# Top-32 attention, soft and top-2 mixture of experts: the first of three strikes of the search moved to ScalarE and TensorE, tiles of a pair staggered

## What is computed

```python
batch, n_heads, seq, head_dim = (4, 8, 576, 64)
scores = scale * np.matmul(q, k.transpose(0, 1, 3, 2))
kth = np.partition(scores, -top_k, axis=-1)[..., -top_k:-top_k + 1]   # top_k = 32
mask = scores >= kth
scores = np.where(mask, scores, -1000000000.0)
scores = scores - np.max(scores, axis=-1, keepdims=True)
attn = np.exp(scores)
attn = attn / (np.sum(attn, axis=-1, keepdims=True) + 1e-09)
return np.matmul(attn, v).astype(np.float32)
```

## Time and profile before

| | |
|---|---|
| runs | 1154.96, 1158.04, 1158.5 us; median 1158.04 |
| the profiled execution | 1157.69 us, of which the span of the instructions is 1155.9 us |
| busy in the span | TensorE 933.9, VectorE 877.4, GpSimd 651.5, ScalarE 416.3 us |
| first and last score search on VectorE | from 7.2 us to about 707.7 us |
| mean granted clock of TensorE | 0.855 of full speed |

### The profile page before, as it was taken

How to read it: one execution, slowest core, us unless ns; L and a number is a source line. 1 busy time by engine, 2 the same in 40 slices (tenths; PEclk the granted TensorE clock), 3 DMA queues, 4 the chain that set the end, 5 groups by cost and what they waited for, 6 DMA issues and landing times.

```text
span 1155.9 us, 18485 instructions
## 1 busy us (share of the span) xinstructions
PE 933.9 (81%) x5335; PEld 721.3 (62%) x5335; DVE 877.4 (76%) x1813; ACT 416.3 (36%) x767; POOL 651.5 (56%) x812
## 2 busy tenths in 40 slices
PE   4777878778888777787777888775779999999995
PEld 3666666566666666666666667322347877778884
DVE  7999999999999999999999996302754344543431
ACT  3444444444444444444444443101244122331110
POOL 2777777777777777777777775100214344444442
PEclk7878787887778888888888787886779999999998
DMA  9811010010010010010110000889923344433232
GB/s 357 354 43 41 3 43 19 23 42 19 23 42 6 37 42 9 33 42 0 42 42 5 37 0 1 321 362 421 425 124 67 83 111 112 111 39 39 39 44 33
DMA packets 21581, 105.06 MB, mean 91 GB/s; under 512 B 2944, under 2 KB 4016, under 8 KB 12464
## 3 DMA queue, kind: packets, MB, share of 16 engines
q1 hardware_dynamic: 13696, 84.53, 18.6%
q0 software_dynamic: 7136, 11.20, 7.4%
q10 hardware_dynamic: 720, 8.98, 2.1%
HBM read 88.35 MB, written 16.07 MB: 90 GB/s over the span
## 4 chain that ended last, share of the span: by engine, by line
issue 39%; DVE 27%; PE 25%; DMA 5%; DVEq 1%; ACT 1%; POOL 1%; SPq 0%; POOLq 0%; ACTq 0%
PE psum L742 11%; DVE arena L913 8%; DVE arena L917 8%; DVE arena L906 5%; PE psum L747 5%; DMA arena<-xs_rows,arena 3%; DMA arena<-w_soft 2%; PE psum L731 2%; PE psum L639 1%; DVE w_lo L1108 1%; PE psum L713 1%; DVE arena L932 1%; PE psum L532 1%; PE psum L620 1%; DVE arena L1083 1%
## 5 line engine op out<-in xcount | busy, mean ns | idle before, releaser
L913 DVE MATCH_REPLACE8 arena<-arena 128x576 f32<-128x576 f32 x432 | 320.2, 755 | 0.0
L917 DVE MAX8 arena<-arena 128x8 f32<-128x576 f32 x432 | 307.4, 760 | 0.0
L499 PE MATMUL psum<-arena 128*128 128x128 f32 x576 | 129.1, 364 | 154.4 <-POOL arena L1197 154.4
L1191 POOL TENSOR_SCALAR arena<-arena 128x576 bf16<-128x576 f32 x142 | 244.6, 1731 | 6.6
L484 PE MATMUL psum<-arena 128*128 128x288 f32 x576 | 220.4, 545 | 4.2 <-DMA arena<-qkv 4.2
L512 PEld LDWEIGHTS psum<-arena 128*128 128x128 f32 (+3 forms) x1600 | 193.4, 182 | 29.7 <-issue 3.3
L512 PE MATMUL psum<-arena 128*128 128x65 f32 (+3 forms) x1600 | 207.4, 271 | 0.9 <-ACT arena L786 0.9
L499 PEld LDWEIGHTS psum<-arena 128*128 128x128 f32 x576 | 81.6, 179 | 186.9 <-POOL arena L1197 161.4
L484 PEld LDWEIGHTS psum<-arena 128*128 128x128 f32 x576 | 152.1, 278 | 52.5 <-DMA arena<-qkv 4.2
L1197 POOL TENSOR_TENSOR arena<-arena 128x576 f32<-128x576 f32 x142 | 178.5, 1278 | 0.0
L785 ACT COPY arena<-psum 128x512 f32<-128x512 f32 x144 | 84.3, 586 | 233.8 <-PE psum L500 233.8
(11 more groups left out here) (177 smaller groups left out, 950.8 us busy)
## 6 DMA issues: line engine op xcount, KB each, us to landing
weights<-w_soft SPq DMA_DIRECT2D x21, 1024.0 KB, 17.3
arena<-qkv SPq DMA_DIRECT2D x15, 1189.0 KB, 5.1
weights<-w_top SPq DMA_DIRECT2D x12, 1024.0 KB, 27.3
arena<-w_soft SPq DMA_DIRECT2D x11, 1024.0 KB, 10.9
weights<-w_top SPq DMA_DIRECT2D x3, 2048.0 KB, 20.9
weights<-w_top ACTq DMA_DIRECT2D x3, 2048.0 KB, 7.7
out<-arena SPq DMA_DIRECT2D x1, 4864.0 KB, 18.4
arena<-w_top SPq DMA_DIRECT2D x4, 1024.0 KB, 27.6
```

The source lines that it names most:

```text
L499: nc.tensor.transpose(bank(4 + t % 2, P, c * P), src[:, c * P:(c + 1) * P], ident)
L913: nc.vector.match_replace(work[t % 2], m8[t % S_SLOTS][:, 8 * r - 8:8 * r], src, NEG) \
L917: nc.vector.max(m8[t % S_SLOTS][:, 8 * r:8 * r + 8], work[t % 2]) \
L1191: nc.gpsimd.tensor_scalar(keep[t % 2], s_sb[t % S_SLOTS], m8[t % S_SLOTS][:, TOPK - 1:TOPK], None, ALU.is_ge) \
```

## The change

For each tile:
- VectorE does four MAX8 and two MATCH_REPLACE8. The first strike is gone from it: ScalarE computes `above` = relu(8th largest - score) from PSUM (bf16), then `hit` = relu(1 - 2^100 * above), which is 1 where a score is at least the 8th largest and 0 elsewhere, and its row sum `n_hit`. Both lie in the tile's `e_sb`, which the exponentials fill later. TensorE then adds hit times -2^126 to the scores in PSUM with two bf16 matmuls (`strike`, weights: the identity times -2^126).
- The second MAX8 and the second strike read those struck scores in PSUM. So the banks of a tile stay in use until that strike (`struck16`), and `qk` of tile t+2 waits for that and no more for the copy.
- With ties the first strike can remove more than 8 scores. So the 32nd value is taken by the count: `sat` is min(n_hit, 32) (a VectorE operation on 128x1), and `select` picks among 25 columns of `m8` the one that belongs to it (an operation on 128x25 with a sum), into `kth_sb`, which the masks now read.
- `qk` contracts 64 partitions: the queries of a head stand in both halves of the partitions, half x holds the keys 288x to 288x+287, and the two matmuls use the two halves of the array's rows. The odd tile takes four matmuls of 64 queries in place of two of 128.
- The work of tiles a and b is listed apart, so that they run half a step shifted, and part of the search of duo n now runs in step n+1. GpSimd's masks run up to a step later.

```diff
+            def qk(j, n, x_, t):
...
+                (pe.wait_ge if w < 2 * NC else partial(hold, pe))(struck16, TPI * j + t + 1)
+                for h, q0, rows in ((w // NC, 0, P),) if w < 2 * NC else ((0, 0, REM), (1, REM, REM)):
                     for x in range(2):
-                        last = nc.tensor.matmul(bank(2 * (t % 2) + x, SH), qT[u][:, w * P:(w + 1) * P],
-                                                kT[u][:, x * SH:(x + 1) * SH], start=True, stop=True)
-                    last.then_inc(scores, 1)
+                        half = slice(HD * x, HD * x + HD)
+                        last = nc.tensor.matmul(bank(2 * (t % 2) + x, SH)[q0:q0 + rows, :],
+                                                qT[u][half, w * P + q0:w * P + q0 + rows],
+                                                kT[u][half, h * SH:(h + 1) * SH], start=True, stop=True,
+                                                skip_group_check=True)
+                last.then_inc(scores, 1)
+            def strike(j, n, x_, t):
...
+                pe.wait_ge(copied, TPI * j + t + 1)
+                pe.wait_ge(hits, TPI * j + t + 1)
+                for x in range(2):
+                    last = nc.tensor.matmul(bank(2 * (t % 2) + x, SH), strike_w, hit[t % S_SLOTS][:, x * SH:(x + 1) * SH],
+                                            start=False, stop=True, skip_group_check=True)
+                last.then_inc(cut, 1)
...
-            steps(pe, [(0, qk), (LAG_O, attn_v), (LAG_T, trans)], lambda m: a_work(early_tiles(m)))
+            steps(pe, [(0, qk_a), (1, strike_b), (LAG_O, attn_v), (0, qk_b), (0, strike_a), (LAG_T, trans)], lambda m: a_work(early_tiles(m)))
...
+            def find_hits(j, n, x, t):
...
+                act.wait_ge(transp, TPI * j + t + 1)
+                act.wait_ge(top8, TPI * j + t + 1)
+                nc.scalar.activation(by_half(above[t % S_SLOTS]), scores_of(t), ACT.Relu,
+                                     bias=m8[t % S_SLOTS][:, 7:8], scale=-1.0).then_inc(relus, 1)
+                act.wait_ge(relus, TPI * j + t + 1)
+                nc.scalar.activation(hit[t % S_SLOTS], above[t % S_SLOTS], ACT.Relu, bias=ones[:, 0:1], scale=STEEP,
+                                     accum_out=n_hit[:, t % S_SLOTS:t % S_SLOTS + 1]).then_inc(hits, 1)
...
-            steps(act, [(0, copy_scores), (LAG_E, exps), (LAG_O, copy_o), (LAG_T, copy_wt)],
+            steps(act, [(0, copy_a), (LAG_E, exp_a), (0, hits_a), (LAG_O, copy_o),
+                        (0, copy_b), (LAG_E, exp_b), (LAG_T, wt_a), (0, hits_b), (LAG_T, wt_b)],
                   lambda m: xT_even(early_tiles(m)))
...
+            def second8(j, n, x, t):
+                hold(dve, cut, TPI * j + t + 1)
+                nc.vector.max(top(t, 1), scores_of(t)).then_inc(top16, 1)
+            def strike16(j, n, x, t):
+                hold(dve, top16, TPI * j + t + 1)
+                nc.vector.match_replace(by_half(work[t % 2]), top(t, 1), scores_of(t), NEG).then_inc(struck16, 1)
...
+            def fourth8(j, n, x, t):
+                slot = t % S_SLOTS
+                nc.vector.tensor_scalar(n_sat[:, slot:slot + 1], n_hit[:, slot:slot + 1], float(TOPK), None,
+                                        ALU.min).then_inc(saturated, 1)
+                hold(dve, struck24, TPI * j + t + 1)
+                nc.vector.max(top(t, 3), work[t % 2]).then_inc(top32, 1)
+            def select(j, n, x, t):
+                slot = t % S_SLOTS
+                dve.wait_ge(saturated, TPI * j + t + 1)
+                hold(dve, top32, TPI * j + t + 1)
+                nc.vector.scalar_tensor_tensor(chosen[x], cst[:, C_KTH:C_KTH + PICKED], n_sat[:, slot:slot + 1],
+                                               m8[slot][:, 7:TOPK], ALU.is_equal, ALU.mult,
+                                               accum_out=kth_sb[:, slot:slot + 1]).then_inc(kth, 1)
...
-            steps(dve, [(0, search_first), (0, search_rest), (LAG_E, mask_last), (LAG_O, recips)],
+            steps(dve, [(1, second_b), (0, first_a), (1, s24_a), (1, s16_b), (1, fourth_a), (1, third_b), (1, select_a),
+                        (0, second_a), (0, first_b), (1, s24_b), (0, s16_a), (LAG_O, recips), (1, fourth_b), (0, third_a),
+                        (1, select_b), (LAG_E, mask_last)],
                   lambda m: xT_odd(early_tiles(m)))
...
-            steps(pool, [(0, neg_max), (LAG_O, o_sums), (LAG_E, mask), (LAG_O, norm)])
+            steps(pool, [(2, mask_b), (2, apply_a), (2, apply_b), (LAG_O, o_sums), (1, mask_a), (0, neg_max), (LAG_O, norm)])
```

More of the change, by code:

```diff
@@ L14 @@
 from contextlib import ExitStack
+from functools import partial
 import concourse.bass as bass
@@ L46 @@
 NEG = -3.0e38
+STRIKE = -2.0 ** 126
+STEEP = -2.0 ** 100
 N, D = B * S, H * HD
@@ L72 @@
 C_BACK = C_LOW + 1
-CW = C_BACK + 1
+C_KTH = C_BACK + 1
+PICKED = TOPK - 7
+CW = C_KTH + PICKED
 M_SAME = 0
@@ L166, in build @@
         zeros = take(D)
+        above = [a[:, 0:S // 2].bitcast(BF16) for a in e_sb]
+        hit = [a[:, S // 2:S].bitcast(BF16) for a in e_sb]
+        strike_w = tiny.bitcast(BF16)
+        n_hit, n_sat, kth_sb = [pos[:, a * S_SLOTS:(a + 1) * S_SLOTS] for a in range(3)]
+        chosen = [list_f[:, a * PICKED:(a + 1) * PICKED] for a in range(2)]
         (w3, wgn_f, so_sb, more, part, slotP_f, ed_f, sm, noise_sb, logit_f, cT_f, soT_f, so4_f, sow, rt_f,
@@ L762, in _ @@
             act.sem_inc(av, 1)
[L764 to L772, removed]
@@ new lines, in exps, with copy_wt @@
+            def exps(j, n, x, t):
+                act.wait_ge(negmax, DPI * j + n + 1)
+                act.wait_ge(copied, TPI * j + t + 1)
+                act.wait_ge(cut, TPI * j + t + 1)
+                nc.scalar.activation(e_sb[t % S_SLOTS], s_sb[t % S_SLOTS], ACT.Exp,
+                                     bias=nmax[n % 3][:, x:x + 1], scale=SCALE).then_inc(expd, 1)
+            def copy_wt(j, n, x, t):
+                if x == 0:
+                    act.wait_ge(av, DPI * j + n + 1)
+                act.wait_ge(transp, TPI * j + t + 1 + S_SLOTS)
+                last = nc.scalar.copy(wT[:, t % 2, 0:NC, :], bank(4 + t % 2).rearrange("p (c q) -> p c q", c=NC))
+                if x == 1:
+                    last = nc.scalar.copy(wT[0:REM, :, NC, :], bank(6, 2 * P)[0:REM, :].rearrange("p (t q) -> p t q", t=2)) \
+                        .then_inc(wt_copied, 1)
@@ L1215, in norm @@
                 last.then_inc(x_done, 1)
-            steps(pool, [(0, neg_max), (LAG_O, o_sums), (LAG_E, mask), (LAG_O, norm)])
+            mask_a, mask_b = each(mask)
+            apply_a, apply_b = each(apply)
+            steps(pool, [(2, mask_b), (2, apply_a), (2, apply_b), (LAG_O, o_sums), (1, mask_a), (0, neg_max), (LAG_O, norm)])
             pool.wait_ge(zeroed, 32)
@@ L1322 @@
     qt = q.transpose(0, 1, 3, 2).reshape(PAIRS, 2, HD, S)
-    for w in range(2 * NC):
-        h, c = w // NC, w % NC
-        qkv[:, HD * h:HD * (h + 1), w * P:(w + 1) * P] = qt[:, h, :, c * P:(c + 1) * P]
-    for h in range(2):
-        first = 2 * NC * P + REM * h
-        qkv[:, HD * h:HD * (h + 1), first:first + REM] = qt[:, h, :, NC * P:S]
-    qkv[:, :, QW:QW + S] = k.transpose(0, 1, 3, 2).reshape(PAIRS, P, S)
+    for x in range(2):
+        rows = slice(HD * x, HD * x + HD)
+        for h in range(2):
+            qkv[:, rows, h * NC * P:(h + 1) * NC * P] = qt[:, h, :, 0:NC * P]
+            first = 2 * NC * P + REM * h
+            qkv[:, rows, first:first + REM] = qt[:, h, :, NC * P:S]
+    kt = k.transpose(0, 1, 3, 2).reshape(PAIRS, 2, HD, 2, SH)
+    qkv[:, :, QW:QW + S] = kt.transpose(0, 3, 2, 1, 4).reshape(PAIRS, P, S)
     vp = v.reshape(PAIRS, 2, S, HD)
```

123 lines of the change are left out of this document (70 added, 53 removed).

## The result

| | before | after |
|---|---|---|
| runs | median 1157.15 us of 4 (1154.96 to 1158.5) | median 1218.72 us of 4 (1218.48 to 1221.98) |
| ratio to before, 95% interval | | **1.0541** [1.0515, 1.0566] |
| profiled execution, span | 1157.69, 1155.9 us | 1221.98, 1220.2 us |
| mean granted clock | 0.855 | 0.774 |
| last full-width search operation ends | 707.7 us | 768.4 us |

The search ends 60.7 us later; behind it, 3.6 us more pass than before. Rather than a forecast gain of 44 us there is a loss of 62.

The account below looks back on a forecast made before the run. VectorE's list was taken to bound the attention: 9.70 - 1.44 + 0.44 + 0.35 = 9.05 us a duo. Over 72 duos 47 us less, 3 more for the ends: 1157.7 - 44 = 1114 us, range 1086 to 1148.

Parts of the forecast that it names:

- TensorE's loop: Strike, hand-overs, scores and second MAX8 in attention: 4.2 us each half duo, 8.4 a duo, below 9.05; clock 0.8 or more.
- the slow rival: Attention paced by the loop through TensorE at low clock: 9.8 us a duo, 1168 us, up to 1219; chance 0.14.
- two hand-overs: Between VectorE and TensorE in each half duo: 0.12 us each, partly an estimate.
- List on VectorE: VectorE's own work in attention: 9.70 - 1.44 + 0.44 = 8.70 us a duo; alone, as a rival, 1089 us, chance 0.22.
- PSUM as source at no cost: Four VectorE operations a duo reading PSUM: cost 0, bounds 0 and 0.045 us an operation; dearer as a rival, chance 0.03.
- `select` waits for GpSimd: On VectorE, `select` has two SBUF inputs and waits for GpSimd's operations: 0.35 us for tile a, 0 for b.
- `sat` waits: Rival on VectorE: `sat` waits too, 0.35 us a duo more, 9.40 a duo, 1139 us; chance 0.15.
- ScalarE hidden: Four more 128x576 passes on ScalarE, 3.1 us a duo, 7.5 of 9.05 in all: hidden by the search, costed at nothing.
- The row halves run side by side: Score matmuls on TensorE's array halves: half the time, 0.53 us a tile; rival of one after the other, chance 0.08.
- The mark set for being wrong: Profile sign: VectorE idle before the second MAX8, released by TensorE, means the loop paces; clock under 0.75, the slow case.

Follow-up runs that it names:

- e2: Kernel before the change with only the scores changed to half height (64 partitions a matmul, two row halves): 1155.76 us, ratio 0.9989.
- e1: Changed kernel with the old full-height scores (128 partitions with zeros, one matmul after the other): 1219.75 us, ratio 1.0534.
- e3: Changed kernel with four of five matmuls of `attn_v` left out, so the output is incomplete: 1179.80 us, ratio 1.0193.
- e7: Changed kernel with six dummy bf16 matmuls of 512 columns a step on TensorE, behind the transposes: 1148.21 us, ratio 0.9914.
- e9: Kernel before the change with 108 semaphore increments more, that nobody waits for, in VectorE's loop body: 1200.96 us, ratio 1.0381.
- e12: Changed kernel with three dummy bf16 matmuls of 512 columns a step on TensorE, behind the transposes: 1147.64 us, ratio 0.9916.
- e10: Changed kernel without `sat` and `select` (threshold from the last column of the sorted maxima) and with six dummy matmuls a step: 1095.10 us, ratio 0.9454.

## Why the prediction was wrong

**The step that failed is the last sentence on TensorE's loop**: "Such idle time shrinks and is split in two, so I expect 0.8 or more". The clock was 0.67. Two things behind it were not seen. The scores at half height lower the clock by themselves (e2), though TensorE is busy for longer. And the argument against the slow rival, that TensorE is busy nearly all the time once its clock is low, was true and didn't bring the clock back in time: in the 18 us from 422 on it was at work for 17.05 and stayed at 1.2 GHz, and the clock came back only behind 442 us, for some 3 us.

**A term was missing in the loop**, and that is the second half of the failed step, for with the clock as forecast (e1, 0.83) but scores that take longer the time is 1219.75 all the same. The sum had VectorE's part, two hand-overs, scores and strike, 4.2 us a half duo, and compared that with 4.5. It left out that `attn_v` stands between the strike of b and the scores of b on TensorE's queue. Before, scores only waited for a copy and had the time of a whole duo; now each waits for a bank that VectorE has just freed. At the full clock that term is hidden (0.56 us of idle time are left behind it), at the low one it isn't: 10.02 us a duo without most of it (e3), 11.4 with it. The slow rival had 9.8, or 1168 us; its upper end, 1219, is the measured time by luck: it took the row halves to run one after the other, which they don't, and had neither `attn_v` nor the stalls.

**A loss that no term covered**: six stalls at the loop's jump, 21 us. I counted what the small operations take on VectorE and not what they add to the length of its loop.

**The balance.** With the clock mostly full, e7 takes 1148. Take its 21.1 us of stalls off: 1127, against the 1114 forecast. In e7 the search ends at 688.1 us rather than 707.7; with the stalls off that is a gain of 40.7 us, where the forecast had 44. Behind the search e7 takes 9.6 us more than the kernel before: 4.4 where the attention drains, with the dummies in it, and 5.9 in the last stage, less 0.7 between. In the last stage the changed kernel too takes 5.7 us more than before (318.7 us from the first `w_lo` of the stage, L1191 at 901.5 us, to the end; before, 313.0 us from 842.95); that was costed at nothing. It isn't shown to be the change's: the same stage takes 318.1 us in e9, which has nothing of the change, and 313.9 in e12, which has all of it. Its cause is open.

**Point by point, the rest.**
- *List on VectorE*, 8.70 a duo without waits, 8.26 without the small operations: measured 8.93 (after, where VectorE never waits) and 8.37 (e10). Good to 0.11 without the small ones; these take 8.93 - 8.37 = 0.56 a duo, forecast 0.44 and a wait of 0.35.
- *PSUM as source at no cost:* 762 ns for MAX8 against 748 and 741 from SBUF, 746 against 741 for the strike. About 0.02 us an operation, inside the bounds. The 62 cycles of the Trainium skill ("VectorE: DVE Perf Modes", TRN2 errata) would be 0.065 each, an estimate by that page's clock of VectorE; the trace doesn't agree for these operations.
- *`select` waits for GpSimd, 0.35 a duo:* it does, in 42 of 144. Those last 315 ns or more, the longest 1010, and each ends some 0.04 us behind one of GpSimd's applies (L1282), as here, where the second apply ends at 415.47 + 2.52 = 417.99 and `select` at 418.02:

```profile
415.47 2.52 POOL L1282 TENSOR_TENSOR arena<-arena 128x576 f32<-128x576 f32 x2
...
417.66 0.36 DVE L987 SCALAR_TENSOR_TENSOR arena<-arena 128x25 f32<-128x25 f32 x1
```

  The others last 217 to 246 ns, and the mean of the 600 us is 267. So 0.04 each, 0.08 a duo, a quarter of the price. The mechanism was right, its size was not.
- *`sat` waits:* no, 136 ns each. The rival falls.
- *ScalarE hidden:* yes in e7 and e10. It was dearer than costed: the sum of the hits is read out by an instruction of its own, 186 ns, once for each tile.
- *The row halves run side by side:* yes. Four records of a tile's scores in 0.76 us at the full clock, 1.33 at the low one; forecast 0.63 and, in the slow rival's sum, 1.1. Strike 0.42 and 0.66; forecast 0.45 and 0.65.
- *The mark set for being wrong*, idle time before the second MAX8 released by TensorE and a clock under 0.75, was the right one: both are there.

## What to carry to other kernels

A change that ties a formerly slack engine into a loop has to be priced at that engine's low clock, with everything that stands in its queue between the loop's steps, and not only with the steps themselves. Fewer rows in a matmul saved nothing here, since the clock fell with them (e2); where the granted clock falls and the engine is in the loop, a few dense dummy matmuls in its queue are a cheap test, and here they were worth 70 us. When instructions are added to a loop that another change has not shortened, look at the jump: idle time there put down to "issue", beside more packets on the instruction queue, points to the loop being fetched anew. That reading rests on the two coming together; no run here takes one without the other.

## What the hardware showed that I had not expected

- The kernel before with half-height scores: clock 0.68 rather than 0.82, with TensorE busy 499.60 us of 600 rather than 472.88.
- 18 us at 1.2 GHz with TensorE busy for 17.05 of them. With three bf16 matmuls of 512 columns more a step the mean granted clock was 0.87 (e12), without them 0.67.
- Stalls of up to 3.7 us at a loop's jump, six in a kernel, with 46 packets of instructions rather than 14; 108 semaphore increments that nobody waits for bring them about in the kernel before (e9).
- A ScalarE operation with a row sum is followed by a read of 186 ns; VectorE's read of the same kind takes 79.
- A short VectorE operation with two inputs from SBUF that begins while GpSimd's apply runs ends with it: 42 of the 43 `select`s that did so, 315 to 1010 ns long rather than 228.
